# At a unit's end: add the attention output first, round x on ScalarE in four pieces, and wait piece by piece

## What is computed

```python
scores = scale * np.matmul(q, k.transpose(0, 1, 3, 2)) + bias.transpose(2, 0, 1)[None, :, :, :]
attn = np.exp(scores - np.max(scores, axis=-1, keepdims=True))
attn = attn / (np.sum(attn, axis=-1, keepdims=True) + 1e-09)
x = np.matmul(attn, v)             # batch 4, heads 8, 576 positions, head size 64
x = x.transpose(0, 2, 1, 3)        # 2304 tokens x 512
h = x @ w_in                       # 512 x 2048
y = (h - np.tanh(h)) @ w_out       # 2048 x 512
g = y @ w_gate; val = y @ w_val    # 512 x 1536 each
out = (g / (1 + np.exp(-g)) * val) @ w_out2
```

## Time and profile before

| | us |
|---|---|
| median of 3 runs | 1268.54 |
| lowest and highest run | 1265.68, 1268.65 |
| the profiled execution, its own time | 1267.85 |
| its span in the profile | 1266.0 |
| TensorE busy | 1198.3 |
| VectorE, ScalarE, GpSimd busy | 635.1, 596.1, 574.0 |
| from the first H of unit 0 to 802 us (middle stage with layer) | 647.36, of which TensorE is busy 639.63 at a granted clock of 1.00 |

### The profile page before, as it was taken

The page is one execution under the profiler, slowest core; times in us unless marked ns, Lnnn a source line. Parts: engine busy times, 40 slices in busy tenths (PEclk is TensorE's granted clock), DMA queues, the critical chain, the costliest instruction groups (busy, mean ns, idle before and its releaser), DMA issues.

```text
span 1266.0 us, 25247 instructions
## 1 busy us (share of the span) xinstructions
PE 1198.3 (95%) x8400; PEld 1132.6 (89%) x8400; DVE 635.1 (50%) x1575; ACT 596.1 (47%) x1300; POOL 574.0 (45%) x664
## 2 busy tenths in 40 slices
PE   5756699999999999999999999999999999999999
PEld 2346699999999999999999999999999999999998
DVE  7967788766666666666666654521211212112111
ACT  6866587655655655655555555521212222122212
POOL 0037689767677676676666644211111111111111
PEclk9978799999999999999999999999999999999999
DMA  4789534344444444444444424400000001000000
GB/s 140 213 231 292 173 98 125 109 140 122 135 120 120 139 120 120 139 120 130 130 120 131 123 90 167 144 26 1 26 26 25 25 14 36 0 25 1 25 1 25
DMA packets 69151, 124.99 MB, mean 99 GB/s; under 512 B 8544, under 2 KB 32096, under 8 KB 69088
## 3 DMA queue, kind: packets, MB, share of 16 engines
q1 hardware_dynamic: 69088, 124.16, 33.3%
HBM read 104.07 MB, written 20.05 MB: 98 GB/s over the span
## 4 chain that ended last, share of the span: by engine, by line
PE 84%; ACT 4%; issue 3%; DVE 3%; POOL 3%; DMA 2%; SPq 1%; POOLq 0%; DVEq 0%; ACTq 0%
PE ps_h L1087 14%; PE ps_y L1106 14%; PE ps_s L1176 12%; PE ps_y L1187 12%; PE ps_s L1040 7%; PE ps_h L1176 6%; PE ps_pt L1176 6%; PE ps_pt L1053 6%; PE ps_pt L1063 5%; PE ps_y L1063 1%; DMA bias_scratch<-x_stage 1%; POOL fr L521 1%; POOL prob L516 1%; ACT wbuf L620 1%; SPq L346 1%
## 5 line engine op out<-in xcount | busy, mean ns | idle before, releaser
L557 POOL TENSOR_TENSOR fr<-x_stage,fr 128x384 fp32r<-128x384 f32 x72 | 73.1, 1015 | 379.9 <-ACT fr L743 379.9
L1106 PE MATMUL ps_y<-fr,wbuf 128*128 128x288 f32 x1536 | 225.4, 295 | 1.1 <-POOL fr L521 0.4
L1087 PE MATMUL ps_h<-fr,wbuf 128*128 128x288 f32 x1440 | 220.1, 296 | 0.7 <-DVE fr L883 0.7
L1106 PEld LDWEIGHTS ps_y<-fr,wbuf 128*128 128x128 f32 x1536 | 210.3, 188 | 2.9 <-POOL fr L521 2.8
L516 POOL TENSOR_SCALAR prob<-prob,rowinv 96x576 f32<-96x576 f32 x192 | 150.7, 791 | 125.5 <-DVE rowinv L851 123.9
L1087 PEld LDWEIGHTS ps_h<-fr,wbuf 128*128 128x128 f32 x1440 | 201.2, 189 | 1.7 <-issue 1.0
L856 DVE TENSOR_TENSOR wbuf<-ps_pt,wbuf 128x480 fp32r<-128x480 f32 x176 | 115.7, 658 | 151.0 <-ACT wbuf L620 150.4
L620 ACT ACTIVATE wbuf<-ps_pt 128x480 fp32r<-128x480 f32 x176 | 100.7, 572 | 185.4 <-PE ps_pt L1053 185.1
L1187 PE MATMUL ps_y<-wbuf,fr 128*128 128x512 f32 x648 | 162.1, 395 | 0.0
L612 ACT ACTIVATE prob<-prob,negmax 96x576 f32<-96x576 f32 x192 | 147.9, 770 | 7.5 <-DVE negmax L841 7.0
L521 POOL TENSOR_TENSOR fr<-g_b,fr 128x288 fp32r<-128x288 f32 x128 | 112.6, 880 | 78.9 <-ACT fr L630 78.9
(11 more groups left out here) (110 smaller groups left out, 1837.4 us busy)
## 6 DMA issues: line engine op xcount, KB each, us to landing
biasb<-bias_scratch SPq DMA_DIRECT2D x192, 216.0 KB, 3.9
k_raw<-k_t SPq DMA_DIRECT2D x63, 288.0 KB, 2.9
v_raw<-v_p SPq DMA_DIRECT2D x64, 160.0 KB, 3.4
q_raw<-q_t SPq DMA_DIRECT2D x64, 144.0 KB, 2.6
w_raw<-w_chunks SPq DMA_DIRECT2D x16, 512.0 KB, 6.3
prob<-w_chunks SPq DMA_DIRECT2D x8, 768.0 KB, 4.2
bias_scratch<-x_stage SPq DMA_DIRECT2D x36, 144.0 KB, 2.5
bias_scratch<-y_stage SPq DMA_DIRECT2D x36, 144.0 KB, 2.5
```

The costliest lines, as they stand in the source:

```text
L1087: mm = eng.matmul(hidden_bank(u, c)[:, 0:T1], w[:, cols], x[:, d, :], start=d == 0 and i == 0, stop=d == KC - 1 and i == 2)
L1106: mm = eng.matmul(ps_y[:, d, 0:T1], w[:, cols], g[c % 2], start=c == 0 and i == 0, stop=c == C1 - 1 and i == 2)
```

## The change

At a unit's end ScalarE runs `o_part` ahead of `g_high`, and then rounds the four chunks of x itself, one instruction each. VectorE gives up `x_high`. It runs `x_out` and `inverse` first and then four `x_low`, one for each chunk. H waits for `x_low` of a chunk ahead of each of its four pieces. `edge` is changed alike.

```diff
+            def x_high(u, c):
+                eng.wait_ge(v_x, u * H + (2 * c + 2))
+                eng.activation(x_hi[:, c, :], x_stage[:, c, :], ACT.Copy).then_inc(a_xhi, 1)
...
+                if pv:
+                    o_part(n - 1, 1 - par, o_bank)
                 if late:
                     g_high(m + 1, 1)
-                if pv:
-                    o_part(n - 1, 1 - par, o_bank)
+                if pv and late:
+                    for c in range(KC):
+                        x_high(moe[0] + 1, c)
...
             def edge():
+                eng.wait_ge(e_score, NQ * (H + 1))
+                for c in range(KC - 1):
+                    x_high(0, c)
                 o_part(H - 1, 1, pt_banks(None)[1])
+                x_high(0, KC - 1)
...
-            def x_high(u, part):
-                wait(eng, v_x, u * H + (H - 2 if part == 0 else H))
-                cs = x_chunks(part)
-                eng.tensor_copy(x_hi[:, cs, :], x_stage[:, cs, :]).then_inc(v_xhi, 1)
-
-            def x_low(u, part):
-                wait(eng, v_xhi, u * 2 + (part + 1))
-                cs = x_chunks(part)
-                eng.tensor_tensor(x_lo[:, cs, :], x_stage[:, cs, :], x_hi[:, cs, :].bitcast(F32), ALU.subtract)\
+            def x_low(u, c):
+                eng.wait_ge(a_xhi, u * KC + (c + 1))
+                eng.tensor_tensor(x_lo[:, c, :], x_stage[:, c, :], x_hi[:, c, :].bitcast(F32), ALU.subtract)\
                    .then_inc(v_xlo, 1)
...
                 if pv and last:
-
-                    x_high(moe[0] + 1, 0)
                     x_out(n - 1, 1 - par, o_bank, x_chunk)
-                    x_low(moe[0] + 1, 0)
-                    x_high(moe[0] + 1, 1)
-                    x_low(moe[0] + 1, 1)
                 if qk and last:
                     inverse(n, par, 2)
+                if pv and last:
+                    for c in range(KC):
+                        x_low(moe[0] + 1, c)
...
             def edge():
-                eng.wait_ge(e_score, NQ * (H + 1))
-                x_high(0, 0)
-                x_low(0, 0)
+                for c in range(KC - 2):
+                    x_low(0, c)
                 x_out(H - 1, 1, pt_banks(None)[1], KC - 1)
-                x_high(0, 1)
-                x_low(0, 1)
+                for c in range(KC - 2, KC):
+                    x_low(0, c)
...
-                        if c == 0:
-                            eng.wait_ge(v_xlo, u * 2 + 1)
-                    if d == KC - 1 and c == 0:
-                        eng.wait_ge(v_xlo, u * 2 + 2)
+                    if c == 0:
+                        eng.wait_ge(v_xlo, u * KC + (d + 1))
```

More of the change, by code:

```diff
@@ L167, in attention_layers_kernel @@
         a_q, v_q, p_khi, p_klo, p_vhi, p_vlo = (sem(x) for x in ("a_q", "v_q", "p_khi", "p_klo", "p_vhi", "p_vlo"))
-        v_xhi, v_xlo = sem("v_xhi"), sem("v_xlo")
+        a_xhi, v_xlo = sem("a_xhi"), sem("v_xlo")
         e_h, a_tanh, v_g, a_ghi, p_glo, e_y, a_y = (sem(x) for x in (
@@ L869, in x_out @@
                 eng.tensor_tensor(dst, bank[rows, 0:T1], x_part[rows, :], ALU.add).then_inc(v_x, 1)
-            def x_chunks(part):
-                return slice(0, KC - 1) if part == 0 else slice(KC - 1, KC)
-            def x_high(u, part):
-                wait(eng, v_x, u * H + (H - 2 if part == 0 else H))
-                cs = x_chunks(part)
-                eng.tensor_copy(x_hi[:, cs, :], x_stage[:, cs, :]).then_inc(v_xhi, 1)
-            def x_low(u, part):
-                wait(eng, v_xhi, u * 2 + (part + 1))
-                cs = x_chunks(part)
-                eng.tensor_tensor(x_lo[:, cs, :], x_stage[:, cs, :], x_hi[:, cs, :].bitcast(F32), ALU.subtract)\
+            def x_low(u, c):
+                eng.wait_ge(a_xhi, u * KC + (c + 1))
+                eng.tensor_tensor(x_lo[:, c, :], x_stage[:, c, :], x_hi[:, c, :].bitcast(F32), ALU.subtract)\
                    .then_inc(v_xlo, 1)
```

## The result

The changed kernel takes 1279.42 us (median of 4 runs, 1277.85 to 1282.74), the kernel before 1267.11 (4 runs beside it, 1265.30 to 1268.65): a ratio of 1.0097, interval 1.0081 to 1.0113. It is 12.3 us slower; the forecast was 1271.1, and the range ended at 1273.0.

The account below looks back on a forecast made before the run. TensorE, busy 1198.3 of 1266.0 us, was taken to bound the kernel. Six ends losing 0.55 each, less 0.1 at the last, gave +3.2 on 1267.85, so 1271.1; the range for 8 in 10 was 1261.5 to 1273.

Parts of the forecast that it names:

- What bounds the kernel, and T0: TensorE bounds; at the ends of units 0 to 5, T0 waits for `x_out`, and the change gains 1.05 us there.
- S1 was the right point to watch: At a unit's end S1 is 1.50 us late, all that can be given back; what is late there stays lost.
- Alternation: At a unit's end the four `x_low` and GpSimd's instructions take turns; S1 at 673.12 instead of 672.57, 0.55 us lost.
- one place: At 165.02 a subtraction issued inside the first of two norms ended at 166.30, and the second norm only then ran.
- the term of 6 x 0.55 = 3.3: At six units' ends the gain at T0 is lost again and 0.55 us more at each.
- rival (c): Chance 0.05: second part of `split_v` also runs ahead of the last `x_low`; 0.7 us for each of six ends, 1275.
- The waits of H: Three more waits in eight H of 128; a wait that is met costs nothing.
- The late `pt_high`: ScalarE's copies delay the next slot's `pt_high` by 0.3 us (bounds 0 and 0.6); this is hidden.
- The edge: At the edge T0's 1.1 us wait for `x_out`, which waits for O, doesn't move; gain 0.
- The last end: At the last unit's end H starts at 753.26 instead of 753.37: gain 0.1 us, at most 0.81.
- (a): Chance 0.35: VectorE keeps the port at units' ends; 0.94 us won at each of six, 5.7 with the last, 1262.1.
- (b): Chance 0.10: some turns are missed, gain at T0 and loss at S1 cancel; 1267.9, within 1.5 us.

Follow-up runs that it names:

- experiment 2: Kernel before with only `o_part` ahead of `g_high` and `x_out` ahead of the casts; casts and two subtractions stay on VectorE: 1268.72 us, ratio 1.0003.
- 8: Changed kernel with `inverse` again behind the four subtractions and `o_part` again behind `g_high`: 1263.83 us against 1267.57 before, ratio 0.9969.
- Experiment 1: Changed kernel with one edit undone, `inverse` of tile 2 again behind the four subtractions: 1264.98 us against 1268.33 before, ratio 0.9974.
- Experiment 10: Changed kernel with the norm over all 128 partitions instead of 96: 1270.00 us against 1268.22 before, ratio 1.0012.
- The small program: Programs in place of the whole computation: a few GpSimd instructions in a row, one or four VectorE subtractions beside them, kinds and partitions varied; total time says nothing.
- experiment 3: Changed kernel with two subtractions and two waits in H instead of four, `inverse` still first: 1282.32 us against 1268.33 before, ratio 1.0097.
- experiment 4: Changed kernel with a wait and a small memset on VectorE that put off the first `x_low`: 1281.98 us against 1268.33 before, ratio 1.0100.
- 7: Changed kernel with two subtractions and two waits in H, and `inverse` behind them: 1265.62 us against 1267.57 before, ratio 0.9977.
- 9: Kernel before with only `inverse` of tile 2 moved ahead of the two subtractions: 1274.24 us against 1267.57 before, ratio 1.0057.

## Why the prediction was wrong

**What bounds the kernel, and T0: right.** T0 waited for `x_out` (experiment 2), not for the norm that the profile names; `o_part` fitted into the hole (678.42, `g_high` kept its place to within 0.1), and T0 came at its natural time. S1 was the right point to watch: the 1.07 won at T0 was lost again by S1 in experiment 2, and 8, without most of it, has the same S1 as 1. The list of waits left one out, `PE ps_pt L1053 <- DVE wbuf L856: 0.9, 1, 0.9`, at 159.59; the change doesn't touch it (0.91 after).

**The step that failed is "Alternation".** The prediction let the first `x_low` in behind norm 1, with norm 2 and `split_g` lengthened, each waiting its turn. It took this from one place, where a subtraction did come in between two norms. In the trace norm 2 and `split_g` passed the waiting `x_low` without any delay, 2.43 us instead of 0.95. What this moved can be counted. The forecast had three of GpSimd's instructions and the first part of `split_v` ahead of the last `x_low`; since the first `x_low` came two instructions late, the second part of `split_v` (L510, 0.95) stands ahead of the third as well. The last `x_low` ended at T0 + 4.52 instead of 3.62, `pt_low` started at 4.55 instead of 3.55, S1 came at 5.93 instead of 4.93. So 1.53 was lost at an end, not 0.55: the term of 6 x 0.55 = 3.3 in the sum measured 6 x 1.52 = 9.1. This is the turn of rival (c), which stood at 0.05 with a price of 0.7 for an end (measured 0.98); its place was right, but the prediction had no mechanism that would bring it about. Experiment 10 shows the cause: with 128 partitions in the norm the first `x_low` has its 0.95, and the kernel takes 1270.0. It isn't the forecast's row of turns to the letter: the second `x_low`, right behind the first, ran at 0.45 ahead of norm 2, and S1 was at 4.59 instead of 4.93.

Why misled: the place is still there in the changed kernel (165.09, two norms 1.90, L816 takes 0.90 between them), beside six ends at which the norm passes. Norm 2 was ready there only when its `rowinv` ended, at 165.48 in the kernel before, 0.46 us into norm 1, and at the ends of the changed kernel 0.14 into it:

```profile
165.32 0.16 DVE L851 RECIPROCAL rowinv<-rowden 96x1 f32<-96x1 f32 x1
```

The small program fits this (passed when the second wait was met early, 0.92 when it was met 0.45 into the first); in the kernel itself that wait wasn't moved alone, and the small programs had turns without a late release too, so for the earlier trace rows it is an explanation that was only argued.

The Trainium skill, "SBUF — State Buffer", section "Who interferes with whom", says that the shared port is an exclusive lock, and that the order of issue, not the shape, decides who blocks. The trace agrees for two instructions (0.95 for a subtraction issued into a norm). It doesn't for the hand-over: norm 2 was issued 0.62 after the waiting `x_low` and went first, and with another shape of the same instruction (128 partitions, experiment 10) it didn't.

**The clock was missing altogether.** No term stood for it; the trace of before holds no fall of the clock at a unit's end. It brought 3.8 of the 12.9 us. At the six ends it came only with waits in H of 1.4 to 2.1 us (the changed kernel, 3 and 4); experiments 1, 2, 7, 8, 9 and 10, whose H waits 1.0 or less there, have none. The length of the wait alone doesn't decide it: the same waits kept the clock at two or three of six ends, and so did 1.6 and 1.7 at the last end of 2, 3 and 7.

**Sizes of the rest.** The waits of H cost nothing, as said (7). The late `pt_high` was hidden, as said. The edge still waits 1.1. The last end was to gain 0.1 and gains nothing: the first copy ended 1.42 after M (764.88 + 0.44) instead of 1.31, and H came 2.42 after M instead of 2.29. Had `g_high` stayed first, 0.6 would have been won there (8).

**The rivals.** (a), a gain of 5.7 us, didn't come: VectorE doesn't keep the port against norm 2. Experiment 1, which keeps norm 2 away, comes nearest: its six ends win 3.8, and its median is 1265.0. That its profiled execution took 1261.1, near the 1262.1 of (a), is luck: it reached the first H of unit 0 at 151.3, 3.3 earlier than the kernel before. (b) is close to experiment 10.

**Still open:** why some instructions over 96 partitions do hand the port over, and why the clock falls at four ends of six (three in experiment 4) with the same waits of TensorE.

## What to carry to other kernels

When an edit moves a small instruction forward, ask what it releases on the other engine, and whether that work shares a port with what now runs beside it: here 0.36 us of `inverse`, ahead of the split instead of behind it, decided between 1265 and 1279 us. A waiting instruction is not sure of the next turn; one row in which it got it is one case, and the prediction's range should hold the case in which the other engine's whole row goes first. And a wait put into the bounding engine can cost more than its length, since the clock may fall behind it.

## What the hardware showed that was not expected

- GpSimd passes a VectorE subtraction that waits at the port: two norms over 96 partitions and `split_g` run at 0.74, 0.74 and 0.79, and the subtraction takes 2.43 instead of 0.45. Over 128 partitions it gets in behind the first (0.68 to 0.95). With 96 it got in, too, in five of fourteen repetitions of the small program.
- VectorE in its turn may run two subtractions behind one another while GpSimd waits (0.95 and then 0.45 in experiment 10); beside subtractions on GpSimd the turns are strict.
- TensorE's granted clock fell from 1.00 to 0.50 for 3.4 us after an idle time of 1.4 to 1.5 us, at four of six like places, at 0.7 to 1.1 us each; and likewise in experiment 3 after 2.0 to 2.1 (at four of six, 1.6 us each). With idle times of 0.3 to 1.0 at these places it never did.
